# Score products of a gated linear attention kernel: one zero-padded product per pair of heads, or one product per head on 64 rows of the array

## The reference

```python
f = 1 / (1 + exp(-f_logit))                       # q, k, v, f_logit: (4, 8 heads, 768, 48)
for t in range(S):
    state = f[:, :, t, :, None] * state + einsum('bhd,bhe->bhde', k[:, :, t], v[:, :, t])
    y[:, :, t] = einsum('bhd,bhde->bhe', q[:, :, t], state)
x = y as (4, 768, 384)
x = x + relu(layernorm(x) * g @ w_ch1) @ w_ch2    # 384 -> 1536 -> 384
h = relu(x @ w_in)                                # 384 -> 1024
out = (h * sigmoid(conv3(h))) @ w_out
```

## Time and profile before

| | |
|---|---|
| median of three runs | 856.74 us (853.94, 856.74, 857.62) |
| span of the profiled execution | 855.1 us, first to last instruction |
| its granted TensorE clock | 0.975 of full speed on average, 1.00 in all windows from 102 to 855 us |
| PE busy | 779.7 us, 91% |
| DVE busy | 624.3 us, 73% |
| ACT busy | 419.1 us, 49% |
| score products, PE busy | 170.4 us in 1152 records |

### The profile page before, as it was taken

The page is one execution under the profiler, slowest core; times in us unless marked ns, Lnnn a source line. Parts: engine busy times, 40 slices in busy tenths (PEclk is TensorE's granted clock), DMA queues, the critical chain, the costliest instruction groups (busy, mean ns, idle before and its releaser), DMA issues. The chain is left out here.

```text
span 855.1 us, 14651 instructions
## 1 busy us (share of the span) xinstructions
PE 779.7 (91%) x5008; PEld 751.9 (88%) x5008; DVE 624.3 (73%) x1425; ACT 419.1 (49%) x900; POOL 191.4 (22%) x203
## 2 busy tenths in 40 slices
PE   3674899989989998999999899899998999999998
PEld 3563889989978997998899899799997999999997
DVE  6985986796688679658867966876245877777775
ACT  3462453336245333624534463451235777777775
POOL 8583241133124114212411430240000000000000
PEclk9776999999999999999999999999999999999999
DMA  6358311342081134207114320210431011111001
GB/s 212 102 141 222 86 70 47 72 115 94 2 186 47 47 82 104 94 2 186 47 48 93 98 88 7 68 47 2 133 99 55 2 56 56 56 55 55 29 1 55
DMA packets 22071, 65.45 MB, mean 77 GB/s; under 512 B 2384, under 2 KB 14160, under 8 KB 22000
## 3 DMA queue, kind: packets, MB, share of 16 engines
q1 hardware_dynamic: 22000, 64.52, 26.8%
HBM read 55.08 MB, written 9.44 MB: 75 GB/s over the span
## 5 line engine op out<-in xcount | busy, mean ns | idle before, releaser
L770 PEld LDWEIGHTS bank<-QZ,K 128*128 128x128 f32 x1152 | 152.7, 203 | 74.3 <-DVE AT L664 37.8
L770 PE MATMUL bank<-QZ,K 128*128 128x128 f32 x1152 | 170.4, 296 | 52.1 <-ACT QZ L502 48.1
L502 ACT COPY QZ<-QP 64x256 f32<-64x256 f32 x288 | 117.4, 408 | 171.7 <-DVE QP L632 167.7
L734 DVE SCALAR_TENSOR_TENSOR HLO<-bank,HHI 128x384 fp32r<-128x384 f32 x96 | 53.5, 557 | 101.5 <-ACT HHI L557 100.8
L1017 DVE SCALAR_TENSOR_TENSOR TB<-HB,CW,TB 128x384 f32<-128x384 f32 x128 | 79.2, 619 | 44.2 <-ACT TB L981 41.9
L557 ACT ACTIVATE HHI<-bank 128x384 fp32r<-128x384 f32 x96 | 47.1, 491 | 124.0 <-PE bank L840 122.6
L838 PE MATMUL bank<-XH,W1H 128*128 128x384 f32 x288 | 103.4, 359 | 2.9 <-issue 2.0
L838 PE MATMUL bank<-HHI,W2H 128*128 128x384 f32 x288 | 103.0, 358 | 0.0
L840 PE MATMUL bank<-XH,W1L 128*128 128x384 f32 x288 | 97.8, 340 | 0.0
L840 PE MATMUL bank<-HHI,W2L 128*128 128x384 f32 x288 | 97.3, 338 | 0.0
L839 PE MATMUL bank<-XL,W1H 128*128 128x384 f32 x288 | 97.2, 338 | 0.0
(11 more groups left out here) (101 smaller groups left out, 1555.0 us busy)
## 6 DMA issues: line engine op xcount, KB each, us to landing
NEAR<-near SPq DMA_DIRECT2D x24, 960.0 KB, 5.0
XB<-x2d SPq DMA_DIRECT2D x8, 577.5 KB, 4.8
X<-w SPq DMA_DIRECT2D x12, 384.0 KB, 4.7
V<-v SPq DMA_DIRECT2D x8, 576.0 KB, 11.5
x2d<-X SPq DMA_DIRECT2D x8, 576.0 KB, 3.8
F<-f SPq DMA_DIRECT2D x14, 288.0 KB, 5.5
Q<-q SPq DMA_DIRECT2D x14, 288.0 KB, 7.6
K<-k SPq DMA_DIRECT2D x14, 288.0 KB, 10.2
```

The source lines that it names most:

```text
L502: ins = nc.scalar.copy(QZ[rows, c, :, par, :].rearrange("p j (n m) -> p j n m", m=m), one)
L770: ins = mm(sb_[slot % 2][:, j * P:(j + 1) * P], K[u.par][:, c, j, :], QZ[:, c, j].rearrange("p a b -> p (a b)"), start=True, stop=True)
```

## The change

Each pair of heads is now two products instead of one: head 0 with rows 0 to 47 of K and QP, head 1 with rows 64 to 111, each with 64 moving columns that are read in place from QP with a stride. The two products write to two different banks, bank 5 for even heads and bank 6 for odd ones, so a slot takes half of both banks and there is no alternation between slots. QZ, its zeroing, `scatter` and the semaphores `qz_zero` and `qz_ready` go. TensorE waits for `prep_ready` of its slot and for the release of the banks by slot s - 1 instead of s - 2. The predicated copy on VectorE is cut into two, one per bank; the copies on ScalarE keep their number and read both banks.

```diff
         bank = [banks[:, i] for i in range(8)]
@@ scalar
-            def scatter(u, slot):
-                st, c = divmod(slot, NC)
-                if slot >= NC or not u.first:
-                    act.wait_ge(score_done, u.count(SLOTS, slot - NC + 1))
-                act.wait_ge(prep_ready, u.count(PREPS, slot + 1))
-                m = 2 << st
-                for par in range(2):
-                    rows = slice(HALF * par, HALF * par + HALF)
-                    one = QP[rows, c].rearrange("p j (n two m) -> p j n two m", two=2, m=m)[:, :, :, 1, :]
-                    ins = nc.scalar.copy(QZ[rows, c, :, par, :].rearrange("p j (n m) -> p j n m", m=m), one)
-                ins.then_inc(qz_ready, 1)
...
-                    scores_of = sb_[slot % 2][:].rearrange("p (h n m) -> p h n m", h=H, m=m)
...
+                of = score_pair[:, :, 0:NP * HALF].rearrange("p par (j n m) -> p j par n m", j=NP, m=m)
+                for n in range(HALF // m):
+                    rows = slice(2 * m * n, 2 * m * n + m)
+                    to = AT[rows, c, :, 2 * m * n + m:2 * m * (n + 1)].rearrange("p (j par) m -> p j par m", par=2)
+                    ins = nc.scalar.copy(to, of[rows, :, :, n, :])
@@ vector, slots 0 to 11
-                dst = AT[:, c].rearrange("p h (n two m) -> p h n two m", two=2, m=m)[:, :, :, 1, :]
...
-                nc.vector.copy_predicated(dst, mask.broadcast_to([P, H, HALF // m, m]),
-                                          sb_[slot % 2][:].rearrange("p (h n m) -> p h n m", h=H, m=m)
-                                          ).then_inc(mask_done, 1)
+                for par in range(2):
+                    dst = AT[:, c, par::2].rearrange("p h (n two m) -> p h n two m", two=2, m=m)[:, :, :, 1, :]
+                    of = sb_[par][:, 0:NP * HALF].rearrange("p (j n m) -> p j n m", j=NP, m=m)
+                    ins = nc.vector.copy_predicated(dst, mask, of)
+                ins.then_inc(mask_done, 1)
@@ tensor
-                pe.wait_ge(qz_ready, u.count(SLOTS, slot + 1))
-                if slot >= MASKED + 2:
-                    pe.wait_ge(copy_done, u.count(COPIED, slot - MASKED - 1))
-                elif slot >= 2:
-                    pe.wait_ge(mask_done, u.count(MASKED, slot - 1))
+                pe.wait_ge(prep_ready, u.count(PREPS, slot + 1))
+                if slot > MASKED:
+                    pe.wait_ge(copy_done, u.count(COPIED, slot - MASKED))
+                elif slot:
+                    pe.wait_ge(mask_done, u.count(MASKED, slot))
...
                 for j in range(NP):
-                    ins = mm(sb_[slot % 2][:, j * P:(j + 1) * P], K[u.par][:, c, j, :],
-                             QZ[:, c, j].rearrange("p a b -> p (a b)"), start=True, stop=True)
+                    for par in range(2):
+                        rows = slice(HALF * par, HALF * par + D)
+                        right = QP[rows, c, j].rearrange("p (n two m) -> p n two m", two=2, m=m)[:, :, 1, :]
+                        ins = mm(sb_[par][:, j * HALF:(j + 1) * HALF], K[u.par][rows, c, j, :], right, start=True, stop=True)
```

More of the change, by code:

```diff
@@ L114, in sem, with phase_a @@
             return ctx.enter_context(nc.semaphore(name))
-        bank = [ctx.enter_context(nc.psum_tensor(f"bank{i}", [P, 512], F32)) for i in range(8)]
+        banks = ctx.enter_context(nc.psum_tensor("bank", [P, 8, 512], F32))
+        bank = [banks[:, i] for i in range(8)]
         X2 = [sb(f"X2_{i}", [P, KT, T]) for i in range(2)]
-        carried = phase_a(nc, sb, sem, bank, X2, q, k, f, v, near, g_ln, w1, w2, x2d, w3, cw, w4)
+        carried = phase_a(nc, sb, sem, bank, banks[:, 5:7], X2, q, k, f, v, near, g_ln, w1, w2, x2d, w3, cw, w4)
         phase_b(nc, sb, sem, bank, X2, x2d, carried, out)
-def phase_a(nc, sbuf, sem, bank, X2, q, k, f, v, near, g_ln, w1, w2, x2d, w3, cw, w4):
+def phase_a(nc, sbuf, sem, bank, score_pair, X2, q, k, f, v, near, g_ln, w1, w2, x2d, w3, cw, w4):
     with ExitStack() as own:
@@ L138, in phase_a @@
         QP = attn("QP", [P, NC, NP, C])
-        QZ = attn("QZ", [P, NC, NP, 2, HALF])
         TOT = {m: attn(f"TOT{m}", [P, NC, NP * C // m]) for m in (2, 4, 8, 16, 32, 64, 128)}
@@ L193, in phase_a @@
         const_ready = sem("const_ready")
-        qz_zero = sem("qz_zero")
         f_ahead, q_ahead, k_ahead = sem("f_ahead"), sem("q_ahead"), sem("k_ahead")
@@ L207, in phase_a @@
         prep_ready = sem("prep_ready")
-        qz_ready = sem("qz_ready")
         score_done = sem("score_done")
@@ L418, in _ @@
             nc.gpsimd.memset(F[0][:, 1:], 0.0).then_inc(pad_f, 1)
-            nc.gpsimd.memset(QZ[:], 0.0).then_inc(qz_zero, 1)
             nc.gpsimd.memset(ID[:], 0.0)
@@ L513, in gates @@
                     nc.scalar.activation(F[u.par][:, c], F[u.par][:, c], ACT.Sigmoid).then_inc(f_ready, 1)
[L515 to L519, removed]
             def near_(u, c):
@@ L526, in score @@
                 st, c = divmod(slot, NC)
-                if slot >= MASKED:
-                    act.wait_ge(score_done, u.count(SLOTS, slot + 1))
-                    m = 2 << st
-                    scores_of = sb_[slot % 2][:].rearrange("p (h n m) -> p h n m", h=H, m=m)
[L532 to L537, removed]
+                if slot < MASKED:
+                    return
+                act.wait_ge(score_done, u.count(SLOTS, slot + 1))
+                m = 2 << st
+                of = score_pair[:, :, 0:NP * HALF].rearrange("p par (j n m) -> p j par n m", j=NP, m=m)
[3 more added lines that the diff above has]
+                    ins = nc.scalar.copy(to, of[rows, :, :, n, :])
+                ins.then_inc(copy_done, 1)
             def ktr(u, c):
@@ L581, in xb @@
                     nc.scalar.copy(nxt.XBH[0][:, d], nxt.XB[0][:, d]).then_inc(nxt.xbh_ready, 1)
-            walk(act, dict(wb=wb, xb=xb, gates=gates, open=open_, near=near_, score=score, ktr=ktr, xnt=xnt, up=up, x2=x2, weights=weights))
+            walk(act, dict(wb=wb, xb=xb, gates=gates, near=near_, score=score, ktr=ktr, xnt=xnt, up=up, x2=x2, weights=weights))
         @block.vector
@@ L661, in score @@
                 m = 2 << st
-                dst = AT[:, c].rearrange("p h (n two m) -> p h n two m", two=2, m=m)[:, :, :, 1, :]
                 mask = MASK[:, st, :].bitcast(I32).rearrange("p (n m) -> p n m", m=m).unsqueeze(1)
-                nc.vector.copy_predicated(dst, mask.broadcast_to([P, H, HALF // m, m]),
-                                          sb_[slot % 2][:].rearrange("p (h n m) -> p h n m", h=H, m=m)
-                                          ).then_inc(mask_done, 1)
+                mask = mask.broadcast_to([P, NP, HALF // m, m])
+                for par in range(2):
[3 more added lines that the diff above has]
+                ins.then_inc(mask_done, 1)
             def lastprep(u, _):
@@ L761, in score @@
                 c = slot % NC
-                pe.wait_ge(qz_ready, u.count(SLOTS, slot + 1))
-                if slot >= MASKED + 2:
-                    pe.wait_ge(copy_done, u.count(COPIED, slot - MASKED - 1))
-                elif slot >= 2:
-                    pe.wait_ge(mask_done, u.count(MASKED, slot - 1))
+                pe.wait_ge(prep_ready, u.count(PREPS, slot + 1))
[3 more added lines that the diff above has]
+                    pe.wait_ge(mask_done, u.count(MASKED, slot))
                 elif not u.first:
-                    pe.wait_ge(xl_ready, u.count(KT, slot - 2))
+                    pe.wait_ge(xl_ready, u.count(KT, -1))
+                m = 2 << slot // NC
                 for j in range(NP):
-                    ins = mm(sb_[slot % 2][:, j * P:(j + 1) * P], K[u.par][:, c, j, :],
-                             QZ[:, c, j].rearrange("p a b -> p (a b)"), start=True, stop=True)
+                    for par in range(2):
+                        rows = slice(HALF * par, HALF * par + D)
+                        right = QP[rows, c, j].rearrange("p (n two m) -> p n two m", two=2, m=m)[:, :, 1, :]
+                        ins = mm(sb_[par][:, j * HALF:(j + 1) * HALF], K[u.par][rows, c, j, :], right, start=True, stop=True)
                 ins.then_inc(score_done, 1)
@@ L776, in ktr @@
                 if c == 0:
-                    pe.wait_ge(copy_done, u.count(COPIED, COPIED - 1))
+                    pe.wait_ge(copy_done, u.count(COPIED, COPIED))
                 else:
```

## The result

The changed kernel takes 970.83 us (median of four, 969.74 to 974.61) against 855.81 (four runs beside it): ratio 1.136, 95% interval 1.134 to 1.139, 115 us slower. The direction was forecast, the size not: 904 us were predicted, 47 us more than before. 982 us, the price of the first rival, lies near the measurement, and its cause is nevertheless not what happened.

A forecast was written before the change was run, and what follows sets the result against it. PE and DVE were taken to bound the kernel together in slots 0 to 12. 856.7 + 0 (products) + 36 (ring) + 3 (first unit) + 8 (entering and leaving) = 904 us; likeliest case 885 to 930, 8-in-10 range 866 to 990.

The forecast's parts named there:

- the first rival: Score products: loads on different rows do not overlap, a slot costs 1.78 us; 982 us in all, chance 0.34. Also Rival 1.
- Products, 0 us: Score products: pairs on separate rows overlap, each as long as a load now; a slot stays at 0.89 us.
- Rival 1: Score products: loads on different rows do not overlap, a slot costs 1.78 us; 982 us in all, chance 0.34.
- The ring: Score banks in loop units: waiting for slot s - 1's copy costs 5.2 us a unit, 36 us in all (0 to 70).
- DVE's waits behind `down` groups: Slots 0 to 11: DVE waits 0.8 us for products behind each of five `down` MLP groups, 4.0 us a unit.
- the two places without a group: Slots 0-1 and 6-7, no MLP group between: 0.3 us each for DVE, PE idle for a copy, 0.8 to 1.4 us.
- Entering and leaving: Switching PE into and out of the 64-row form at each slot: 8 us taken, of 0 to 78.
- The clock, rival 4: Clock drops where PE idles longest, slot 1: 3 us x 7, so 925 us; chance included in the forecast's 0.46.
- The first unit: Unit before the loop: products show beside prep in half of 12 slots; plus 3 us, from -8 to +16.
- The QZ hop: Two copies between prep and products go: up to 0.87 us less per wait, in the loop 3.4 us in all.

The follow-up runs named there:

- e2_one_slot: Kernel before, with one edit: a slot waits for the copy of slot s - 1; banks still alternate, QZ and 128-row products stay. 907.33 us, ratio 1.062.
- e1_two_pairs: Changed kernel with a second pair of banks, so a slot waits for slot s - 2 again; part of the result is wrong. 856.42 us, ratio 1.0015.
- e9_spread_fill: Changed kernel with 18 instead of 15 MLP groups spread over the slots, plus unused filling products ahead of slot 1. 937.83 us, ratio 1.095.
- e8_slot_fill: Kernel before with the wait for slot s - 1, plus 14 unused filling products ahead of slot 1 in loop units. 898.24 us, ratio 1.050.

## Why the prediction was wrong, step by step

- **Products, 0 us.** Right. Eight pairs in 0.97 us, as eight single loads before. A load of 48 rows takes as long as one of 128; what saves is that two run at once. Rival 1 had the time and not the cause.
- **The ring, 36 us for seven units.** The cause was right: DVE waits for products, PE idles at slots 1, 7 and 13. Alone and at full clock it measured 27.4 us in the loop. That the total is near is in part luck, for the split was wrong. I gave 4.0 of the 5.2 us a unit to DVE's waits behind `down` groups, and 0.6 to the two places without a group, with PE idle for 0.8 to 1.4 us. In e2_one_slot DVE's waits come to 12.4 us in the whole loop, 1.8 a unit, and PE idles 2.59 and 1.70 us at the two places; in the changed kernel it is 2.67 and 3.25. I had let PE wait for one copy, but HLO and a prep stand before that copy. These stretches are also what the clock falls behind.
- **Entering and leaving, "I take 8 us" of 0 to 78.** This is the first failed size: the rung is 37.4 us, most of it by the edges' own count (at most 15 x 7 x 0.35 = 37). I counted on the empty pipeline ahead of a slot and on waits that would cover it. In fact PE goes into 71 of the 84 slots between two groups without a wait in the changed kernel, and each of those at full clock takes 1.59 us instead of 1.24, both edges in full. The Trainium skill (TensorEngine Tiling (Array Packing), section Key Properties) says that changing the tiling mode drains TensorE; I cited the sentence and gave it a fifth of its price. The runs agree with it: the first 48-row load starts 0.43 us after the load ahead, about when the product ahead ends, and in and out cost 0.35 us.
- **The clock, rival 4.** Second failed size, and a fault of method: I named the mechanism, priced it at 21 us at slot 1 only, and left it out of the sum. It measured 32.2 us in the loop. With idle stretches of 2.67 and 3.25 us in each unit it was part of the forecast case, not a rival.
- **The first unit, 3 us of -8 to +16.** 14.6 us. I let half of the preps cover the products, but with the wait for slot s - 1 copy and product follow each other in every slot, and the products are slow there:

```profile
20.94 0.78 DVE L644 COPY_PREDICATED AT<-MASK,bank 128x256 f32<-128x256 int32 x1
21.51 0.78 DVE L607 TENSOR_TENSOR K<-K,TOT 128x256 f32<-128x256 f32 x1
21.83 1.81 PEld L753 LDWEIGHTS bank<-QP,K 48*128 48x128 f32 x16 [1.66 <-issue]
```

  The sixteen loads take some 1.8 us, 1.2 GHz, in all 18 slots of the first unit, where five of the kernel before took 0.97 at full clock. The low clock alone does not cost it: e1_two_pairs has it in all 18 slots too and needs 91.0 us. With the ring it does, and that the weights' DMA hides it was wrong: e2_one_slot loses 13.8 us there.
- **The QZ hop.** Counted inside the ring and not beside it. In the changed kernel no run shows it alone. Without the ring it shows: in e1_two_pairs PE's idle time in the loop falls from 29.0 to 5.7 us, and the edges take what that gives.

Sum with the measured sizes: 0 + 27.4 + 37.4 + 32.2 + 14.6 + 1.3 = 112.9 instead of 47, in the order of the ladder. A loop unit takes 87.9 us, where 79 to 81 was to show the forecast right and 89 to 90 rival 1. The range held the time (866 to 990) only because it had been stretched to rival 1, and that is luck.

## What to carry to other kernels

A form that writes two banks at once halves the depth of the PSUM ring: ask first which engine lags and how much slack the ring gives it, here one slot of DVE's work. Alternating between full-row and 64-row products costs about 0.35 us per excursion here, so short runs of small products woven into large ones are the wrong place for it. Try two such changes in both orders: alone, the form cost nothing, because it filled waits that the ring's second slot had left; with the ring it cost 37 us. And idle stretches like the 2.67 and 3.25 us here, which a new wait brings into an otherwise dense stream, belong into the sum twice, once as idle time and once as lower clock behind them.

## What the runs showed of the hardware

- Products on rows 0 to 47 and 64 to 111 into two banks, issued alternately, overlap fully: 16 loads of 48 x 128 in 0.97 us. Grouped by half they overlap only in part: 1.47 us.
- A change between 128-row and 64-row products holds back the next load until about the end of those in flight: 0.35 us for in and out in the changed kernel, and visible with one single added product per slot.
- 196 useless products made a kernel 32.6 us faster, by keeping the granted clock at 0.99 instead of 0.93.
- The clock also fell where PE never idled longer than 1.22 us (e9_spread_fill, 13.7 us at half clock behind slot 17), and stayed up behind idle stretches of 1.70 us (e8_slot_fill).
- The window figure of the clock can miss: it says 1.00 for the first 103.5 us after the change, while the loads there run at half pace.
